# One of three quads of feature rows moved from VectorE to GpSimd in 20 bias blocks

## What is computed

```python
rel = pos[:, None] - pos[None, :]                       # 576 x 576
x = (log1p(abs(rel)) / log1p(maximum(pos[:, None], 1)))[..., None]
h = maximum(x @ w1 + b1, 0.0)                           # 32 hidden features
bias = h @ w2                                           # 8 heads
scores = scale * q @ k.T + bias
attn = softmax(scores)
h = maximum(x_tokens @ w1[e], 0.0); out += p[:, e] * (h @ w2[e])   # 4 experts
```

## Time and profile before

| | |
|---|---|
| runs | 618.24, 616.42, 618.50 us; median 618.24 |
| profiled execution | 619.06 us, span 617.2 us |
| PE | 581.0 us busy, 94% of the span |
| DVE | 296.1 us, 48% |
| ACT | 262.7 us, 43% |
| POOL | 119.7 us, 19% |
| mean granted TensorE clock | 0.981 |

### The profile page before, as it was taken

One profiled execution on the slowest core, in us unless ns is written; L12 is line 12 of the kernel. 1 busy time (PEld: TensorE's weight loads), 2 busy tenths in 40 slices (PEclk: granted clock), 3 DMA queues, 4 the chain that ended last, 5 costly groups with the idle time before them and its releaser, 6 DMA issues.

```text
span 617.2 us, 9758 instructions
## 1 busy us (share of the span) xinstructions
PE 581.0 (94%) x3864; PEld 468.1 (76%) x3864; DVE 296.1 (48%) x608; ACT 262.7 (43%) x506; POOL 119.7 (19%) x176
## 2 busy tenths in 40 slices
PE   3857998979999999999999999999999999999997
PEld 1325666636678878878888788998899889889986
DVE  6925776679535543365334633362254226224511
ACT  4645666487626644365344643252045015303400
POOL 5124888100001135231342311000000000000000
PEclk9966999989999999999999999999999999999999
DMA  4773665187372723465152311341233014122201
GB/s 149 200 276 116 192 193 147 69 237 218 116 235 65 236 84 89 111 184 160 36 171 87 119 35 70 103 137 34 69 84 121 35 35 139 66 69 60 79 35 51
DMA packets 60654, 72.72 MB, mean 118 GB/s; under 512 B 23232, under 2 KB 39872, under 8 KB 60608
## 3 DMA queue, kind: packets, MB, share of 16 engines
q1 hardware_dynamic: 60416, 72.08, 38.4%
q10 hardware_dynamic: 192, 0.01, 0.0%
HBM read 59.10 MB, written 12.98 MB: 117 GB/s over the span
## 4 chain that ended last, share of the span: by engine, by line
PE 84%; DMA 4%; ACT 4%; DVE 3%; issue 2%; POOL 2%; SPq 0%; ACTq 0%; DVEq 0%; POOLq 0%
PE m_bank L1095 12%; PE scores L1078 11%; PE x_bank L1095 11%; PE m_bank L1078 10%; PE scores L1095 10%; PE x_bank L1078 9%; PE turn L1029 5%; PE scores L1000 4%; PE scores L1058 4%; PE scores L968 3%; DMA bias_scratch<-rows 3%; PE x_bank L1058 3%; PE turn L968 2%; PE turn L1033 1%; DVE hidden L679 1%
## 5 line engine op out<-in xcount | busy, mean ns | idle before, releaser
L627 POOL TENSOR_SCALAR probs<-probs,recip 128x576 f32<-128x576 f32 x72 | 53.2, 749 | 234.0 <-DVE recip L714 233.7
L730 DVE TENSOR_TENSOR w_lo<-w_raw,w_hi 128x1024 fp32r<-128x1024 f32 x64 | 80.4, 1256 | 21.1 <-ACT w_hi L885 21.1
L699 DVE CUSTOM_DVE_ANT_0 probs<-scores,bias 128x576 f32<-128x576 f32 x72 | 51.9, 754 | 49.5 <-PE scores L1000 37.6
L869 ACT COPY probs_t<-turn 128x512 f32<-128x512 f32 (+2 forms) x80 | 42.4, 551 | 68.8 <-PE turn L1029 67.6
L885 ACT CAST w_hi<-w_raw 128x1024 fp32r<-128x1024 f32 x64 | 66.6, 1045 | 0.2 <-DMA w_raw<-w_in 0.2
L863 ACT ACTIVATE probs<-probs,neg_max 128x576 f32<-128x576 f32 x72 | 55.4, 772 | 26.6 <-DVE neg_max L699 26.6
L1029 PE MATMUL turn<-ident,probs 128*128 128x128 f32 x288 | 45.2, 285 | 3.4 <-POOL probs L627 3.3
L1078 PE MATMUL scores<-x_hi,w_hi 128*128 128x384 f32 (+2 forms) x148 | 47.8, 323 | 0.0
L1078 PE MATMUL scores<-x_lo,w_hi 128*128 128x384 f32 (+2 forms) x148 | 47.3, 319 | 0.0
L1078 PE MATMUL scores<-x_hi,w_lo 128*128 128x384 f32 (+2 forms) x148 | 47.2, 319 | 0.0
L1078 PE MATMUL m_bank<-x_hi,w_hi 128*128 128x512 f32 (+2 forms) x124 | 44.9, 362 | 0.0
(11 more groups left out here) (138 smaller groups left out, 1256.8 us busy)
## 6 DMA issues: line engine op xcount, KB each, us to landing
w_raw<-w_in SPq DMA_DIRECT2D x64, 512.0 KB, 3.5
qk_raw<-qk_t_in SPq DMA_DIRECT2D x16, 576.0 KB, 4.5
bias<-bias_scratch SPq DMA_DIRECT2D x16, 576.0 KB, 4.8
bias_scratch<-rows SPq DMA_DIRECT2D x16, 288.0 KB, 5.3
v<-v_in SPq DMA_DIRECT2D x32, 128.0 KB, 3.3
bias_scratch<-probs_t SPq DMA_DIRECT2D x10, 288.0 KB, 3.0
out_dram<-acc SPq DMA_DIRECT2D x8, 256.0 KB, 2.0
bias_scratch<-probs SPq DMA_DIRECT2D x5, 288.0 KB, 3.0
```

Source lines behind the costliest of these rows:

```text
L627: pool.tensor_scalar(tile, tile, recip[:, stat(f, p, j)], 1.0, ALU.mult, ALU.mult).then_inc(normed, 1)
L699: dve.tensor_tensor_reduce(probs_of(f, p, j).rearrange("p (c j) -> p c j", c=2), score_of(f, j)[:, :, 0:HALF], bias_of(f, p, j).rearrange( ...
L730: dve.tensor_tensor(lo, raw, hi.bitcast(F32), ALU.subtract).then_inc(w_lo_out, 1)
L869: act.copy(sub_out(f, p, i), sub_in(n, i)).then_inc(out_act, 1)
```

## The change

In blocks 16 to 35 quad 2 is made by GpSimd instead of DVE, with the same TENSOR_SCALAR, into the same buffer. DVE makes quads 0 and 1, ACT quad 3. GpSimd has a semaphore of its own, `hid_pool`, and `sum_block` waits for it as a further condition. GpSimd's 20 instructions stand between its two groups of `normalise`, each behind the same wait that DVE and ACT have (`turned` and `maxed` for blocks 16 and 17, `hid_used` for the rest).

```diff
@@ -287,6 +287,10 @@
+        def quads_on_dve(n):
+
+            return ON_DVE if n < EARLY else ON_DVE - 1
@@ -641,6 +645,21 @@
+                def hidden_of_block(n):
+                    if n >= EARLY + 2:
+                        pool.wait_ge(hid_used, n - 1)
+                    elif n % 2:
+                        pool.wait_ge(maxed, blk(0, 5, 3) + 1)
+                    else:
+                        pool.wait_ge(turned, turn_n(0, 6, 4) + 1)
+                    quad = ON_DVE - 1
+                    group = QUADS * n + quad
+                    pool.tensor_scalar(hidden(n, quad), window(group), shift[:, group:group + 1], 0.0,
+                                       ALU.add, ALU.max).then_inc(hid_pool, 1)
+
+                for n in range(EARLY, BLOCKS):
+                    hidden_of_block(n)
                 for at in range(SLOTS * PAIRS):
@@ -674,7 +693,7 @@
-                    for quad in range(ON_DVE):
+                    for quad in range(quads_on_dve(n)):
@@ -962,7 +981,9 @@
-                    pe.wait_ge(hid_dve, ON_DVE * (n + 1))
+                    pe.wait_ge(hid_dve, sum(quads_on_dve(o) for o in range(n + 1)))
+                    if n >= EARLY:
+                        pe.wait_ge(hid_pool, n - EARLY + 1)
```

More of the change, by code:

```diff
@@ L257, in attention_and_experts @@
         table_ready, shift_ready, w2_steps = sem("table_ready"), sem("shift_ready"), sem("w2_steps")
-        hid_dve, hid_act, hid_used, scaled = (
-            sem(s) for s in ("hid_dve", "hid_act", "hid_used", "scaled"))
+        hid_dve, hid_act, hid_pool, hid_used, scaled = (
+            sem(s) for s in ("hid_dve", "hid_act", "hid_pool", "hid_used", "scaled"))
         rows_stored = [sem(f"rows_stored{r}") for r in range(ROW_RING)]
```

## The result

The changed kernel takes 621.82 us in the median of 6 runs (619.81 to 623.25), the kernel before 617.34 us (615.92 to 618.50, 6 runs). The ratio is 1.0068, with a 95% interval of 1.0047 to 1.0090. The forecast was no change, 618.0 us with a range up to 619.8.

What follows compares the result with a forecast made beforehand. PE was taken as the bound from 133 us on. About 0.2 us won by the end of sum 21, all else nothing, gave 618.9 us profiled from 619.06, or 618.0 against the median 618.24; range 616.0 to 619.8.

Steps and rivals of the forecast that it cites:

- What bounds the kernel: PE bounds from 133 us on; before that it stops 1.63 us ahead of sum 18, 2.53 ahead of sum 20.
- A quad is added on GpSimd: Each of 20 quads in blocks 16 to 35 costs GpSimd 0.75 us, priced from `normalise`; upper end 1.41 us.
- The turns with DVE: GpSimd and DVE alternate by instruction; at position 1 sum 20 comes 0.06 us later, sum 21 0.25 us earlier.
- Rival 3: GpSimd's quad takes 1.41 us and holds DVE; PE waits at sums 18 to 21 and later: 620.0 to 622.7 us, 8 in 100.
- turning point: GpSimd quad price, 0.94 us, from which the slow-quad case was said to decide, by the 0.38 us left at block 26.
- Further positions: After 133 us the quads cost nothing if PE's expert matmuls cover them; uncovered, 0.3 us for each of positions 3 to 5.
- The fourth wait: One more wait at each of 20 sums: nothing for 18, up to 0.05 us for two; upper bound 3.0 us.
- The clock: PE's low clock after the rest before sum 20 was kept in the forecast; holding the upper level would give 1.81 us.
- a stop of PE at a sum after 21: Sign of a wrong forecast: PE stopping at any sum later than 21.
- undisturbed quads of 0.75 us: Sign of a right forecast: GpSimd's quads read 0.75 us where nothing hinders them.

Runs made afterwards that it cites:

- run with DVE's quads first: Kernel before, no quad on GpSimd; at positions 0 and 1 DVE makes the next two blocks' quads ahead of `w_lo`: 617.15 us against 617.58, ratio 0.9991.
- run with multiplies: Changed kernel with GpSimd's quad made by two multiplies in place of add and max, output not valid: 617.92 us against 618.09, ratio 1.0004.
- run with blocks 18 to 21: Changed kernel with GpSimd's quad in blocks 18 to 21 only, the others made as before: 620.53 us, ratio 1.0039.
- price table: Kernel before with 15 further GpSimd instructions of various operations on 128x576 numbers, four times over, behind GpSimd's last work: one run, 617.13 us.
- run with blocks 24 to 35: Changed kernel with GpSimd's quad in blocks 24 to 35 only, blocks 16 to 23 made as before: 619.36 us against 618.09, ratio 1.0024.

## Why the prediction was wrong

- **What bounds the kernel.** Right. PE from 133 us on, and sums 18 to 21 ahead of it. That DVE's quads, not ACT's as the label said, were last at sum 20 is shown by the run with DVE's quads first (0.67 us at sum 20, 0.98 at sum 21).
- **"A quad is added on GpSimd", 0.75 us.** This is the step that failed. I took the price of `normalise` because form, shape and operand kinds agree, and I bounded it above by a subtraction of 1.41 us. The operations decide: add and max take 2.22 us, outside both ends. Two multiplies in the same place bring 0.75 us and the old time back. No row before showed a maximum on GpSimd, and I drew the upper end from the dearest row there was, as if it were the dearest that the engine has.
- **The turns with DVE.** Right for a cheap quad, to 0.1 us at sums 20 and 21 in the run with multiplies. It would have been wrong for the quad as it is: a slow instruction on GpSimd does not hold `w_lo` longer than a cheap one does (below).
- **Rival 3, GpSimd's quad is slow.** Its premise is what happened, with 8 in 100, and its two places were right: sums 18 to 21, and a stop at later positions. Its mechanism was not. It had DVE held for longer at every turn and PE waiting for DVE's quads; PE waited for GpSimd's own quads, which follow one another, while DVE's were over 0.9 us before them at sums 18 and 20. It worked out 620.0 to 622.7 us with a quad of 1.41 us; that the measured 621.82 lies inside, with a quad of 2.2, is luck: its quad was too cheap and its hold on DVE too long. Its turning point, 0.94 us, rests on the same turns, and no run has a price between 0.75 and 2.2.
- **Further positions, "cost: nothing".** Right for a quad of 0.75 us (25.12 us from sum 24 to sum 34 in the run with multiplies, 25.10 before), wrong at 2.2: 0.82 us in the profile.
- **The fourth wait.** Nothing that can be told, as taken: all 20 are there in the run with multiplies, and its interval leaves 1.2 us for them together, 0.06 each.
- **The clock.** I kept it as it was. It got 1.33 us dearer in the profiled execution, behind stops of PE of 1.91, 1.20, 1.84 and 1.20 us between sums 17 and 21. The run with blocks 18 to 21 has the same four stops (1.21 for the second) and nearly the same stretch behind them, 6.90 us from sum 21 to sum 22 (6.98 in the changed kernel). That the stops are the cause is not shown: the same stop went with either level of the clock (below).
- **The range.** It ended at 619.8, just short of the 620.0 at which rival 3 begins, because the price was trusted.

The prediction had named a stop of PE at a sum after 21 as a sign of being wrong, and undisturbed quads of 0.75 us as a sign of being right. The profile has the stop (0.2 us at sum 25) and not the quads.

## What to carry to other kernels

An instruction moved to another engine has to be priced with its own operations: the same form on the same shape took from 0.75 to 2.28 us here. Where no row has the operation, the dearest neighbour is no upper bound, and a lone probe in an idle stretch of the engine costs one run. Before moving work off a late engine, look at what stands in front of it in its own list: the order of DVE, ACT and the loads gave 2.4 us where GpSimd cost 4.5, and each step forward has to be followed to the load that it delays.

## What the runs showed of the hardware

- GpSimd's TENSOR_SCALAR on 128x576 fp32 has a cheap form, 0.747 us, for mult and mult, mult and add, add and mult. Every other pair tried took 2.2 to 2.3 us, and a single add or maximum 1.66 to 1.73. A multiply by 1.0 behind an add makes it 2.3 times faster. The Trainium skill (GPSIMD Engine Reference, Performance versus the Vector engine) gives 1.8 cycles per element as the best case, an estimate of 0.86 us; the trace is below it for the cheap pairs and far above for the rest.
- A slow GpSimd instruction holds a `w_lo` on DVE no longer than a cheap one of the same shape. In the run with multiplies a quad of 0.75 us started 0.10 us ahead of a `w_lo`, which took 0.48 more than its usual 1.23. In the price table subtract and mult, 2.22 us long, started 0.11 ahead of another and cost it the same 0.48:

```profile
131.59 0.75 POOL L658 TENSOR_SCALAR probs<-table,shift 128x576 f32<-128x576 f32 x1 [2.28 <-PE scores L989]
131.69 1.71 DVE L749 TENSOR_TENSOR w_lo<-w_raw,w_hi 128x1024 fp32r<-128x1024 f32 x1 [0.19 <-ACT w_hi L904]
...
401.87 2.22 POOL L679 TENSOR_SCALAR probs<-table,shift 128x576 f32<-128x576 f32 x1
401.98 1.71 DVE L763 TENSOR_TENSOR w_lo<-w_raw,w_hi 128x1024 fp32r<-128x1024 f32 x1 [0.45 <-ACT w_hi L918]
```

  Both times the hold ended 0.6 us after GpSimd's start (0.10 + 0.48, 0.11 + 0.48). In the changed kernel a `w_lo` that began 0.37 behind a quad's start (140.26) took 1.45, held to the same 0.6, and one that began 1.90 behind (a quad from 124.04 to 126.44) took its usual time:

```profile
125.94 1.23 DVE L749 TENSOR_TENSOR w_lo<-w_raw,w_hi 128x1024 fp32r<-128x1024 f32 x1 [0.24 <-ACT w_hi L904]
```

  In the changed kernel GpSimd's quads beside DVE's work took up to 3.46 us in place of 2.20, and two quads on DVE took 1.33 to 1.81 us beside GpSimd's, in place of 0.94. The Trainium skill (SBUF — State Buffer, SBUF: two separate sides) says that the one that comes second stands still for the whole instruction. The cheap quads come near that, 0.6 of 0.75 us; the slow ones do not, 0.6 of 2.22.
- The clock does not follow from the length of a stop alone. The run with blocks 24 to 35 has the same stop of 2.53 us ahead of sum 20 as the earlier trace rows, and its sum 21 ran at the upper level, 1.18 us in place of 2.15. In the run with the price table, which is the kernel before at this place, the same stop of 2.53 us was followed by the lower level already at sum 20 (2.15 us).

```profile
130.61 1.18 PE L989 MATMUL scores<-probs,w_block 128*32 128x288 f32 x16 [2.53 <-ACT bias L857]
131.90 1.18 PE L989 MATMUL turn<-bias,w_block 128*32 128x288 f32 x16
```
